# Seven half-block products in place of eight in the last matrix product, with the sums of blocks on POOL and VectorE

## The chip, the cores and the metric

The kernel runs on one core of one Trainium2 chip. The metric is the device time of one execution in microseconds (us); the lower the better. Three runs of the kernel before took 679.25, 680.24 and 680.92 us, median 680.24 us.

## The reference, cut to what matters

Three layers follow each other: attention with keys and values pooled by 8, a soft mixture of experts, and a dense layer with a squared-relu gate. The change touches only the last one, which makes 4608 x 512 outputs from a hidden width of 2048:

```python
def _moe2_ref(x, w_in, w_out, s, b):
    h = x @ w_in                  # 4608x512 @ 512x2048
    r = np.maximum(h, 0.0)
    g = s * (r * r) + b
    return (g @ w_out)            # 4608x2048 @ 2048x512
```

The input x of this layer is c @ slot_out with 32 slots, so the kernel first folds slot_out into w_in (the matrix g_st, 128 rows) and gets h from g_st and the transposed routing weights cT with one matmul of 128 rows.

## The kernel before, in words

All operands are float32. The last product is made in fp32r (one pass of TensorE over a float32 operand) with both factors split into a high and a low part: g_hi*w_hi + g_hi*w_lo + g_lo*w_hi. So each product of blocks is three matmuls.

The tokens go in 9 chunks of 512 (CHUNKS, CH); the hidden width in 16 parts f of 128 (F2C). One chunk and one f is a unit, and there are 144 of them. Per unit:

- TensorE, `hidden`: one matmul of 512 columns into bank 4 or 5 (L1451), issued AHEAD = 3 units early.
- ScalarE, `relu`: bank to r_sb (L845); ScalarE, `high`: g_sb plus b, rounded to fp32r, to r2_hi (L854).
- VectorE, `gate`: s*r*r to g_sb (L1093); VectorE, `low`: g_sb + b - r2_hi to r2_lo (L1099). Both have all their tensor inputs in SBUF.
- TensorE, `products`: for 4 tiles of 128 tokens three matmuls of 512 columns each (L1467, L1468, L1469), accumulated over f in four PSUM banks.

Each engine has its own queue and works it off in order; the order is written out in `units` for ScalarE (L863) and VectorE (L1109), and in `products` (L1454) for TensorE. Waits are on counting semaphores: `low` of unit u lets `products` of unit u start (lo_ready), the end of `products` of u-2 lets `high` of u write its buffer again (unit_done), and `relu` of a unit lets TensorE use that bank again (r_ready). In `units`, ScalarE does relu(f+1), then high(f), and VectorE gate(f+1), then low(f). In the first chunk these queues also make the split of w_out: ScalarE w_hi (L830), VectorE w_lo (L1085), one f each unit; and `keep_g` (L838, L1079). After each chunk four tiles of 128x512 are copied to o_sb (`finish`, L861 and L1107, two on each engine) and stored by SyncE's queue (L644).

POOL (GpSimd) works in the attention stage only: it pools keys and values (L664, L671, L677) and normalises (L684). Its last instruction is a memset at L698.

```python
                    for m in range(MT):
                        toks = slice(P * m, P * (m + 1))
                        acc = acc_bank(odd, m)[:, :]
                        pe.matmul(acc, r2_hi[:, f % 2, toks], w_hi[:, f, :], start=(f == 0), stop=False)
                        pe.matmul(acc, r2_hi[:, f % 2, toks], w_lo[:, f, :], start=False, stop=False)
                        last = pe.matmul(acc, r2_lo[:, f % 2, toks], w_hi[:, f, :], start=False, stop=(f == F2C - 1))
```

Of the kernel before, what the change touches and what calls it, by code (L numbers as in the profile page):

```python
# [18 lines left out]
def pooled_attention_soft_moe_squared_relu_kernel(  # L19
# [55 lines left out]
    AHEAD = 3  # L75
# [18 lines left out]
    assert GL * GH == KEYS and DEN <= BANK and F1 == 2 * BANK and F2 == 4 * BANK and N % CH == 0 and CHUNKS % 2 == 1  # L94
# [3 lines left out]
    with ctx:  # L98
# [15 lines left out]
        early = sb("early", [P, WO, MAT])  # L114
# [42 lines left out]
        r2_hi = sb("r2_hi", [P, 2, CH], F32R)  # L157
        r2_lo = sb("r2_lo", [P, 2, CH], F32R)
# [48 lines left out]
        G_B = (6, 7)  # L207

        def acc_bank(c_odd, m):

            return bank[G_B[m] if c_odd and m < 2 else m]


        TILE_ORDER = (2, 3, 0, 1)
# [86 lines left out]
        h_ready = sem("h_ready")  # L301
        g_ready = sem("g_ready")
        r_ready = sem("r_ready")
# [3 lines left out]
        acc_ready = sem("acc_ready")  # L307
        o_dve = sem("o_dve")
        o_act = sem("o_act")
        stored = [sem(f"stored{m}") for m in range(MT)]  # L310

# [214 lines left out]

        block = ctx.enter_context(nc.Block())

        @block.sync
        def _(sp):
# [103 lines left out]

            for c in range(CHUNKS):
                for n, m in enumerate(TILE_ORDER):
                    sp.wait_ge((o_dve, o_act)[n % 2], 2 * c + n // 2 + 1)
                    sp.dma_start(tile_rows(MT * c + m), o_sb[:, m, :]).then_inc(stored[m], 16)  # L644
            for m in range(MT):
                sp.wait_ge(stored[m], 16 * CHUNKS)

        @block.gpsimd
        def _(pool):
# [48 lines left out]
            pool.memset(hT[:, :, :, :], 0.0).then_inc(hT_zero, 1)  # L698

        @block.scalar  # L700
        def _(act):
# [124 lines left out]
            def split(f):  # L826

                act.wait_ge(wout_in[f // (F2C // WO)], 16)
                wv = early[:, f // (F2C // WO), :].rearrange("p (c f) -> p c f", f=D)
                act.activation(w_hi[:, f, :], wv[:, f % (F2C // WO), :], ACT.Copy).then_inc(w_hi_ready, 1)  # L830

            def keep_part(n):
                act.wait_ge(g_part_psum, n + 1)
                act.activation(g_part[n], bank[n][:, :], ACT.Copy).then_inc(g_part_kept, 1)
# [5 lines left out]
            def relu(n, u, before):  # L840
# [4 lines left out]
                act.activation(r_sb[:, n % 2, :], bank[4 + n % 2][:, :], ACT.Relu).then_inc(r_ready, 1)  # L845

            def high(n, u, c, first):

                act.wait_ge(g_ready, u + 1)
                if n >= 2:  # L850
                    act.wait_ge(unit_done, c * (F2C - 1) + (n - 1))
                elif not first:
                    act.wait_ge((unit_done, acc_ready)[n], c * (F2C - 1, MT)[n])
                act.activation(r2_hi[:, n % 2, :], g_sb[:, n % 2, :], ACT.Identity, bias=sb_col[:, 1:2]).then_inc(hi_ready, 1)  # L854

            def finish(c, odd, second, m):

                act.wait_ge(acc_ready, c * MT + (m + 1))
                if not second:
                    act.wait_ge(stored[m], c * 16)  # L860
                act.activation(o_sb[:, m, :], acc_bank(odd, m)[:, :], ACT.Copy).then_inc(o_act, 1)  # L861

            def units(c, odd, first, second, final):  # L863

                for f in range(F2C):
                    if not (final and f == F2C - 1):
                        relu(f + 1, c * F2C + (f + 1), not first or f)
                    high(f, c * F2C + f, c, first)
                    if first and f + 1 < F2C:
                        split(f + 1)  # L870
                    if first and f < 2:
                        keep_g(2 + f)
                    if not first and f in (0, 2):
                        finish(c - 1, not odd, second, TILE_ORDER[1 + f])

# [7 lines left out]
            relu(0, 0, False)  # L883
            split(0)
            units(0, False, True, False, False)
            units(1, True, False, True, False)
            with act.Fori(2, CHUNKS - 1, 2) as c:
                units(c, False, False, False, False)
                units(c + 1, True, False, False, False)
            units(CHUNKS - 1, False, False, False, True)  # L890
            finish(CHUNKS - 1, False, False, TILE_ORDER[1])
# [3 lines left out]
        def _(dve):  # L895
# [192 lines left out]
            def gate(n, u, before):  # L1088

                dve.wait_ge(r_ready, u + 1)  # L1090
                if before:
                    dve.wait_ge(lo_ready, u - 1)
# [434 lines left out]
```

## Time and profile before

| what | value |
|---|---|
| median of the runs shown | 680.24 us (679.25 to 680.92) |
| the profiled execution | 681.13 us, span 679.3 us |
| TensorE busy | 646.2 us (95%), 5170 matmuls |
| VectorE busy | 369.3 us (54%) |
| ScalarE busy | 325.4 us (48%) |
| POOL busy | 114.8 us (17%) |
| first of the `products` matmuls | 250.8 us |
| last of the `products` matmuls | 674.3 us |

The span is the stretch of the trace from the first to the last instruction; 1.8 us of the profiled execution lie around it. In the trace a matmul's recorded duration includes its way through the array, and matmuls overlap, so what a matmul costs is the distance from its start to the next one's start, not its duration. PE is TensorE's matmuls, PEld its weight loads (each matmul has one, and it runs beside the matmul before). DVE is VectorE, ACT ScalarE, POOL GpSimd.

### The profile page before, as it was taken

To read this page: it belongs to the slowest core of one execution; us is meant where nothing else is said; L and a number is where in the kernel's file an instruction comes from. 1 tells how busy PE (TensorE), PEld (TensorE's weight loads), DVE (VectorE), ACT (ScalarE), POOL (GpSimd) and SP (SyncE) were. 2 spreads that over 40 slices of the span, in tenths; PEclk is the share of its full clock that TensorE was granted. 3 is DMA by queue.
4 is the path that set the end of the run, shared out by engine and by line. 5 is a ranking of instruction groups with operands and counts; after the bars stand their busy time and mean duration, and the time that the engine had idled before them with its cause. 6 is when DMAs were issued, how large, how long until landed. Compare 5 with 4: busy or idle time off the path is not lost.

```text
span 679.3 us, 13164 instructions
## 1 busy us (share of the span) xinstructions
PE 646.2 (95%) x5170; PEld 501.3 (74%) x5170; DVE 369.3 (54%) x610; ACT 325.4 (48%) x599; POOL 114.8 (17%) x117
## 2 busy tenths in 40 slices
PE   6787999989998889999999999999999999999997
PEld 6565677767653248888888888888888888888885
DVE  5757575646344747664454454554544554545543
ACT  1576777767421165654344444443444434443442
POOL 3799777622210000000000000000000000000000
PEclk8899999989999999999999999999999999999999
DMA  9688959573489930010010010000000100100101
GB/s 339 223 264 301 357 201 404 172 295 127 156 311 429 425 166 1 1 52 11 1 62 1 1 62 0 25 37 0 31 31 0 62 0 0 62 1 0 63 0 63
DMA packets 25233, 80.45 MB, mean 118 GB/s; under 512 B 6496, under 2 KB 14688, under 8 KB 22368
## 3 DMA queue, kind: packets, MB, share of 16 engines
q1 hardware_dynamic: 25184, 79.76, 31.5%
q8 instruction: 35, 0.57, 0.4%
q14 instruction: 14, 0.11, 0.1%
HBM read 70.32 MB, written 9.44 MB: 117 GB/s over the span
## 4 chain that ended last, share of the span: by engine, by line
PE 83%; DMA 8%; POOL 3%; DVE 2%; issue 2%; ACT 1%; ACTq 0%; SPq 0%; DVEq 0%; POOLq 0%
PE bank L1467 19%; PE bank L1469 19%; PE bank L1468 19%; PE bank L1451 5%; DMA late<-in_moe_w_dram 4%; PE bank L1318 4%; DMA kvbuf<-in_k_dram 3%; PE bank L1305 2%; PE bank L1242 2%; PE bank L1275 2%; PE bank L1401 2%; PE bank L1348 2%; POOL kvbuf L664 1%; PE bank L1364 1%; PE bank L1201 1%
## 5 line engine op out<-in xcount | busy, mean ns | idle before, releaser
L1467 PE MATMUL bank<-w_hi,r_hi 128*128 128x512 f32 x576 | 224.4, 389 | 1.4 <-DVE r_lo L1099 1.4
L1468 PE MATMUL bank<-w_lo,r_hi 128*128 128x512 f32 x576 | 224.2, 389 | 0.0
L1469 PE MATMUL bank<-w_hi,r_lo 128*128 128x512 f32 x576 | 224.2, 389 | 0.0
L1093 DVE SCALAR_TENSOR_TENSOR win_sb<-win_sb,sb_col 128x512 f32<-128x512 f32 x144 | 108.4, 753 | 197.6 <-ACT win_sb L845 197.5
L845 ACT ACTIVATE win_sb<-bank 128x512 f32<-128x512 f32 x144 | 86.2, 598 | 217.7 <-PE bank L1451 217.7
L1467 PEld LDWEIGHTS bank<-w_hi,r_hi 128*128 128x128 f32 x576 | 108.1, 188 | 24.4 <-DVE r_lo L1099 2.0
L1469 PEld LDWEIGHTS bank<-w_hi,r_lo 128*128 128x128 f32 x576 | 108.1, 188 | 22.4
L1468 PEld LDWEIGHTS bank<-w_lo,r_hi 128*128 128x128 f32 x576 | 108.1, 188 | 22.4
L1099 DVE SCALAR_TENSOR_TENSOR r_lo<-win_sb,sb_col,r_hi 128x512 fp32r<-128x512 f32 x144 | 107.6, 747 | 1.5 <-ACT r_hi L854 1.5
L854 ACT ACTIVATE r_hi<-win_sb,sb_col 128x512 fp32r<-128x512 f32 x144 | 103.3, 717 | 1.6 <-PE bank L1469 1.6
L1451 PE MATMUL bank<-cT,g_st 128*128 (+1 forms) x144 | 56.4, 393 | 0.0
L802 ACT ACTIVATE aT<-bank 72x512 f32<-72x512 f32 x72 | 38.8, 588 | 28.0 <-PE bank L1318 28.0
L684 POOL TENSOR_TENSOR ex<-ex,den 128x576 f32<-128x576 f32 x36 | 41.4, 1150 | 49.4 <-DVE den L998 49.3
L1318 PE MATMUL bank<-ident,ex 128*72 128x128 f32 x288 | 39.6, 281 | 8.0 <-POOL ex L684 5.5
L1318 PEld LDWEIGHTS bank<-ident,ex 128*72 128x72 f32 x288 | 29.5, 116 | 21.5 <-issue 13.7
L948 DVE TENSOR_REDUCE mx<-bank 128x8 f32<-128x576 f32 x36 | 27.2, 756 | 29.6 <-PE bank L1242 24.5
L664 POOL TENSOR_TENSOR kvbuf<-kvbuf 128x768 f32<-128x768 f32 x18 | 32.7, 1817 | 14.1 <-DMA kvbuf<-in_v_dram 8.0
L707 ACT ACTIVATE qT<-bank 128x512 f32<-128x512 f32 x36 | 21.5, 597 | 22.6 <-PE bank L1275 22.4
L1451 PEld LDWEIGHTS bank<-cT,g_st 128*128 128x128 f32 x144 | 27.0, 188 | 6.6 <-DVE g_st L1079 0.8
L1275 PE MATMUL bank<-ident,qbuf 128*128 128x128 f32 x144 | 23.4, 286 | 4.3 <-DMA qbuf<-in_q_dram 3.1
L987 DVE TENSOR_REDUCE den<-ex 128x8 f32<-128x584 f32 x36 | 27.1, 752 | 0.0
L994 DVE TENSOR_TENSOR ex<-bank,mx 128x576 f32<-128x576 f32 x36 | 26.9, 748 | 0.0
(131 smaller groups left out, 552.3 us busy)
## 6 DMA issues: line engine op xcount, KB each, us to landing
early_third<-in_moe_w_dram SPq DMA_DIRECT2D x6, 2048.0 KB, 14.1
kvbuf<-in_k_dram SPq DMA_DIRECT2D x12, 768.0 KB, 5.5
kvbuf<-in_v_dram SPq DMA_DIRECT2D x12, 768.0 KB, 6.2
out_dram<-win_sb SPq DMA_DIRECT2D x36, 256.0 KB, 2.4
qbuf<-in_q_dram SPq DMA_DIRECT2D x8, 1024.0 KB, 9.1
early<-in_moe_w_dram SPq DMA_DIRECT2D x4, 2048.0 KB, 12.4
late<-in_moe_w_dram SPq DMA_DIRECT2D x4, 2048.0 KB, 20.2
win_sb<-in_moe_w_in_dram SPq DMA_DIRECT2D x4, 1024.0 KB, 5.3
```

Of the source, the lines that this page charges most:

```text
L664: pool.tensor_tensor(buf[:, :, 0:ROW // 2], buf[:, :, 0:ROW // 2], buf[:, :, ROW // 2:ROW], ALU.add).then_inc(pool_step, 1)
L684: pool.tensor_tensor(e, e, r, ALU.mult).then_inc(a_ready, 1)
L802: act.activation(aT[:, HB * g:HB * (g + 1), :], bank[A_B[g]][0:KEYS, :].rearrange("p (a g) -> p a g", a=HB), ACT.Copy).then_inc(aT_kept, 1)
L845: act.activation(r_sb[:, n % 2, :], bank[4 + n % 2][:, :], ACT.Relu).then_inc(r_ready, 1)
L854: act.activation(r2_hi[:, n % 2, :], g_sb[:, n % 2, :], ACT.Identity, bias=sb_col[:, 1:2]).then_inc(hi_ready, 1)
L1093: dve.scalar_tensor_tensor(out=g_sb[:, n % 2, :], in0=r_sb[:, n % 2, :], scalar=sb_col[:, 0:1], in1=r_sb[:, n % 2, :], op0=ALU.mult, op1=A ...
L1099: dve.scalar_tensor_tensor(out=r2_lo[:, n % 2, :], in0=g_sb[:, n % 2, :], scalar=sb_col[:, 1:2], in1=r2_hi[:, n % 2, :].bitcast(F32), op0= ...
L1318: last = pe.transpose(bank[A_B[g]][0:KEYS, P * a:P * (a + 1)], ex[:, U % EXR, HB * g + a, 0:KEYS], ident[:, :])
L1451: pe.matmul(bank[4 + f % 2][:, :], g_st[:, P * f:P * (f + 1)], cT[:, bass.ds(c * CH, CH)], start=True, stop=True).then_inc(h_ready, 1)
L1467: pe.matmul(acc, r2_hi[:, f % 2, toks], w_hi[:, f, :], start=(f == 0), stop=False)
L1468: pe.matmul(acc, r2_hi[:, f % 2, toks], w_lo[:, f, :], start=False, stop=False)
L1469: last = pe.matmul(acc, r2_lo[:, f % 2, toks], w_hi[:, f, :], start=False, stop=(f == F2C - 1))
```

## The change

The first 512 tokens are still made as before ("easy" units, with the f in the order FORDER, and the matmuls of `hidden` issued with a lead that grows from 1 to 3 units). The other 4096 tokens go in 16 halves of 256 tokens (HALVES). In a half, the f are taken in pairs k and k+8: a step works on a 2x2 matrix of blocks (two tiles of 128 tokens, two parts of 128 of the hidden width) times a 2x2 matrix of blocks of w_out (two parts f, left and right 256 columns). It needs seven products of 128x128 by 128x256 in place of eight, three matmuls each. A half has 8 steps, so there are 128 steps.

Per step:

- TensorE: two matmuls of 256 columns for h (`hidden`, both into bank 7), issued 5 steps ahead; 21 matmuls of 256 columns (`steps`).
- ScalarE: relu of 512 columns; `add_b` (Identity with bias, 512 columns, in place); `high` (Copy, 896 columns).
- POOL: `token_sums`: three tensor_tensor instructions of 256, 128 and 128 columns, each waiting for the one before; all inputs in SBUF.
- VectorE: `gate` of 512 columns; `low` as a subtraction of 896 columns, both inputs in SBUF; and for 7 of 8 steps a `join` of 256 columns that puts the half before together from the seven sums in PSUM.

The seven sums of a half take 256 columns each (half_bank). ScalarE copies the first to SBUF (keep_p1, once a half). The output is stored as before, one DMA of 256 KB for each 128 tokens.

The block sums of w_out (4 combinations for each of 8 k) are made during the first chunk: POOL makes them (`combos`, 4 instructions of 256 columns for each k), ScalarE rounds them (`combos_high`, 1024 columns, 8 times), and POOL (k < 4) or VectorE (k >= 4) makes the low part (`combos_low`, 1024 columns).

The core of the diff:

```diff
+    AHEAD = 5
+    FORDER = (0, 1, 2, 3, 4, 8, 5, 9, 6, 10, 7, 11, 12, 13, 14, 15)
...
+        def lead(u):
+
+            return 1 if u < 6 else 2 if u < 9 else 3
...
 @block.gpsimd
+            def combos(k):
+
+                if k >= 2:
+                    pool.wait_ge(t_hi_ready, k - 1)
+                    if k - 2 < KP // 2:
+                        pool.wait_ge(t_lo_pool, k - 1)
+                    else:
+                        pool.wait_ge(t_lo_dve, k - 1 - KP // 2)
+                pool.tensor_tensor(t_raw_of(k, T1), raw_block(k, 0, 0), raw_block(k, 0, 1), ALU.subtract).then_inc(t_made, 1)
+                pool.tensor_tensor(t_raw_of(k, T3), raw_block(k, 1, 1), raw_block(k, 0, 1), ALU.add).then_inc(t_made, 1)
+                pool.wait_ge(t_made, COMBOS * k + 1)
+                pool.tensor_tensor(t_raw_of(k, T6), raw_block(k, 1, 1), t_raw_of(k, T1), ALU.subtract).then_inc(t_made, 1)
+                pool.wait_ge(t_made, COMBOS * k + 3)
+                pool.tensor_tensor(t_raw_of(k, T4), raw_block(k, 1, 0), t_raw_of(k, T6), ALU.subtract).then_inc(t_made, 1)
...
+            def token_sums(n, c, k):
+
+                a = a_sb[:, n % ARING, :]
+                pool.wait_ge(gate_ready, c * KP + (k + 1))
+                pool.tensor_tensor(a[:, 4 * P:6 * P].rearrange("p (x f) -> p x f", x=2), a[:, P:3 * P].rearrange("p (x f) -> p x f", x=2),
+                                   a[:, 0:P].unsqueeze(1).to_broadcast([P, 2, P]), ALU.subtract).then_inc(s_made, 1)
+                flip = slice(5 * P, 6 * P)
+                pool.wait_ge(s_made, c * (3 * KP) + (3 * k + 1))
+                pool.tensor_tensor(a[:, 6 * P:7 * P], a[:, P:2 * P], a[:, flip], ALU.add).then_inc(s_made, 1)
+                pool.wait_ge(s_made, c * (3 * KP) + (3 * k + 2))
+                pool.tensor_tensor(a[:, 7 * P:8 * P], a[:, 6 * P:7 * P], a[:, 3 * P:4 * P], ALU.subtract).then_inc(s_made, 1)
...
 @block.scalar
+            def high(n, c, k, first):
+
+                act.wait_ge(s_made, c * (3 * KP) + 3 * (k + 1))
+                if first and k == 1:
+                    act.wait_ge(acc_ready, MT)
+                else:
+                    act.wait_ge(*done_two_before(c, k))
+                act.activation(hi_sb[:, n % 2, :], a_sb[:, n % ARING, P:2 * CH], ACT.Copy).then_inc(hi_ready, 1)
...
+            begun = 1
+            high_at = {3: 0, 5: 1, 7: 2, 8: 3, 9: 4, 11: 5, 14: 6, 15: 7}
+            for u in range(F2C):
+                while begun <= u + lead(u):
+                    relu(begun, begun, bank[4 + begun % 2] if begun < F2C else bank[7], begun >= 2)
+                    begun += 1
+                high_easy(u)
+                if u + 2 >= F2C:
+                    add_b(u + 2, u + 2)
+                if u + 1 < F2C:
+                    split(FORDER[u + 1])
+                if u < 2:
+                    keep_g(2 + u)
+                if u in high_at:
+                    combos_high(high_at[u])
...
 @block.vector
+            def low(n, u):
+
+                dve.wait_ge(hi_ready, u + 1)
+                dve.tensor_tensor(lo_sb[:, n % 2, :], a_sb[:, n % ARING, P:2 * CH], hi_sb[:, n % 2, :].bitcast(F32),
+                                  ALU.subtract).then_inc(lo_ready, 1)
...
+            def steps(c, odd, first, final):
+
+                for k in range(KP):
+                    n = KP * odd + k
+                    low(n, step(c, k))
+                    if not (final and k >= KP - 3):
+                        gate(n + 3, step(c, k) + 3, True)
+                    if first and k in (0, 1):
+                        keep_tile(2 * k + 1)
+                    if not first and k < PARTS7:
+                        join(c - 1, 1 - odd, k)
...
 @block.tensor
+            def products():
+                issued = 3
+                for u in range(F2C):
...
+                    while issued <= u + lead(u) + 2:
+                        hidden_at(issued)
+                        issued += 1
...
+            def steps(c, odd, first, second, final):
...
+                    for at, lhs, rhs_hi, rhs_lo in half_blocks(k):
+                        acc = half_bank(odd, at)
+                        opens = k == 0 and (at == AT1 or at % 2 == 1)
+                        hi, lo = (t[:, n % 2, P * lhs:P * (lhs + 1)] for t in (hi_sb, lo_sb))
+                        pe.matmul(acc, hi, rhs_hi, start=opens, stop=False, skip_group_check=True)
+                        pe.matmul(acc, hi, rhs_lo, start=False, stop=False, skip_group_check=True)
+                        last = pe.matmul(acc, lo, rhs_hi, start=False, stop=(k == KP - 1), skip_group_check=True)
```

## Rows read from the trace of the kernel before

**Rows 1.** The page: slices of TensorE, its granted clock and POOL; the chain.

```profile
PE   6787999989998889999999999999999999999997
POOL 3799777622210000000000000000000000000000
PEclk8899999989999999999999999999999999999999
...
PE bank L1467 19%; PE bank L1469 19%; PE bank L1468 19%; PE bank L1451 5%; DMA late<-in_moe_w_dram 4%; PE bank L1318 4%; DMA kvbuf<-in_k_dram 3%; PE bank L1305 2%; PE bank L1242 2%; PE bank L1275 2%; PE bank L1401 2%; PE bank L1348 2%; POOL kvbuf L664 1%; PE bank L1364 1%; PE bank L1201 1%
```

**Rows 2.** Stretches of the last layer: busy (count) of PE, PEld, DVE, ACT, POOL; clock.

```profile
250.80:298.10 47.30, 47.30 (x209) 39.19 (x210) 33.73 (x50) 26.84 (x48) 0.00 (x0) 1.00 0.00 1
298.10:674.50 376.40, 376.40 (x1662) 311.61 (x1660) 189.10 (x269) 160.90 (x269) 0.00 (x0) 1.00 0.06 23
```

**Rows 3.** Timeline, one unit, hidden to hidden: start, us, engine, line.

```profile
400.97 0.39 PE L1451 MATMUL bank<-cT,g_st 128*128 x1
401.20 0.39 PE L1467 MATMUL bank<-w_hi,r_hi 128*128 128x512 f32 x1
401.40 0.60 ACT L845 ACTIVATE win_sb<-bank 128x512 f32<-128x512 f32 x1 [1.74 <-PE bank L1451]
401.89 0.72 ACT L854 ACTIVATE r_hi<-win_sb,sb_col 128x512 fp32r<-128x512 f32 x1
402.03 0.75 DVE L1093 SCALAR_TENSOR_TENSOR win_sb<-win_sb,sb_col 128x512 f32<-128x512 f32 x1 [1.53 <-ACT win_sb L845]
402.70 0.75 DVE L1099 SCALAR_TENSOR_TENSOR r_lo<-win_sb,sb_col,r_hi 128x512 fp32r<-128x512 f32 x1
...
403.92 0.39 PE L1451 MATMUL bank<-cT,g_st 128*128 x1
```

**Rows 4.** Timeline, runs of matmuls with loads of 128 columns, fp32 (two passes) and transposes.

```profile
174.57 0.53 PEld L1201 LDWEIGHTS bank<-ident 128*128 128x128 f32 x4
174.60 0.69 PE L1201 MATMUL bank<-ident 128*128 128x128 f32 x4
...
211.76 1.97 PE L1409 MATMUL bank<-fold,scratch 128*128 128x32 f32 x16 [0.69 <-ACT scratch L815]
...
247.31 1.88 PE L1446 MATMUL bank<-scratch,fold 128*128 128x512 f32 x4
```

**Rows 5.** Weight loads of the last layer, grouped by line.

```profile
L1468 PEld LDWEIGHTS bank<-w_lo,r_hi 128*128 128x128 f32 x576 | 108.1, 188 | 22.4
```

**Rows 6.** ScalarE and VectorE, groups by line and shape.

```profile
L819 ACT ACTIVATE cT<-bank 128x512 fp32r<-128x512 f32 x8 | 4.8, 597 | 17.0 <-PE bank L1390 17.0
L819 ACT ACTIVATE cT<-bank 128x128 fp32r<-128x128 f32 x4 | 1.1, 276 | 0.0
...
L1065 DVE TENSOR_TENSOR cT<-bank,cT 32x512 fp32r<-32x512 f32 x16 | 11.0, 690 | 11.7 <-ACT cT L819 11.3
L1065 DVE TENSOR_TENSOR cT<-bank,cT 32x128 fp32r<-32x128 f32 x8 | 2.3, 290 | 0.2
```

**Rows 7.** Timeline, start of the first chunk: ScalarE, and the first product.

```profile
248.86 0.72 ACT L854 ACTIVATE r_hi<-win_sb,sb_col 128x512 fp32r<-128x512 f32 x1
249.49 0.61 ACT L830 ACTIVATE w_hi<-early 128x512 fp32r<-128x512 f32 x1
250.00 0.75 DVE L1099 SCALAR_TENSOR_TENSOR r_lo<-win_sb,sb_col,r_hi 128x512 fp32r<-128x512 f32 x1
250.01 0.58 ACT L838 ACTIVATE g_st<-bank 128x512 fp32r<-128x512 f32 x1
...
250.80 0.50 PE L1467 MATMUL bank<-w_hi,r_hi 128*128 128x512 f32 x1 [1.38 <-DVE r_lo L1099]
```

**Rows 8.** POOL, groups by line and shape.

```profile
L671 POOL TENSOR_TENSOR kvbuf<-kvbuf 128x384 f32<-128x384 f32 x18 | 18.0, 1000 | 0.2
L677 POOL TENSOR_TENSOR vp<-kvbuf 128x192 f32<-128x192 f32 x22 | 12.6, 591 | 0.9
```

**Rows 9.** Timeline, a VectorE copy within SBUF beside POOL, and one with POOL idle.

```profile
16.32 1.81 POOL L664 TENSOR_TENSOR kvbuf<-kvbuf 128x768 f32<-128x768 f32 x1 [5.06 <-DMA kvbuf<-in_v_dram]
17.24 1.04 DVE L916 COPY vp<-vp 128x192 f32<-128x192 f32 x1
18.21 0.99 POOL L671 TENSOR_TENSOR kvbuf<-kvbuf 128x384 f32<-128x384 f32 x1
...
196.15 0.23 DVE L1025 COPY sT<-scratch 128x128 f32<-128x128 f32 x1
```

**Rows 10.** VectorE beside POOL, groups by line: all 36 of each.

```profile
L987 DVE TENSOR_REDUCE den<-ex 128x8 f32<-128x584 f32 x36 | 27.1, 752 | 0.0
L994 DVE TENSOR_TENSOR ex<-bank,mx 128x576 f32<-128x576 f32 x36 | 26.9, 748 | 0.0
```

More of the change, by code:

```diff
@@ new lines, in _ @@
+            pool.wait_ge(matrix_used, LAST_SLOT + 1)
+            for i in range(WO):
+                pool.wait_ge(wout_in[i], 16)
+            for k in range(KP):
+                combos(k)
+                if 1 <= k <= KP // 2:
+                    combos_low(k - 1)
+            pool.wait_ge(t_hi_ready, KP)
+            pool.wait_ge(t_lo_dve, KP // 2)
+            for k in range(KP):
+                token_sums(k, 0, k)
+            with pool.Fori(1, HALVES - 1, 2) as c:
+                for x in range(2):
+                    for k in range(KP):
+                        token_sums(KP * x + k, c + x, k)
@@ L700, in _ @@
+            for k in range(KP):
+                token_sums(k, HALVES - 1, k)
         @block.scalar
@@ L838, in keep_g, with relu @@
                 act.activation(g_block(n, slice(0, P)), g_found(n, slice(0, P)), ACT.Copy).then_inc(g_hi, 1)
-            def relu(n, u, before):
+            def relu(n, u, h_bank, before):
                 act.wait_ge(h_ready, u + 1)
@@ L856, in finish @@
-            def finish(c, odd, second, m):
-                act.wait_ge(acc_ready, c * MT + (m + 1))
-                if not second:
[L860 to L874, printed above, removed]
+                a = a_sb[:, n % ARING, 0:CH]
@@ new lines, in keep_tile, with keep_p1 @@
+            def keep_tile(m):
+                act.wait_ge(acc_ready, m + 1)
+                act.activation(o_sb[:, m, :], bank[ACC_B[m]][:, :], ACT.Copy).then_inc(o_act, 1)
+            def keep_p1(c, odd, second):
+                act.wait_ge(half_ready, c * PARTS7 + (AT1 + 1))
+                if not second:
+                    act.wait_ge(joined, c * PARTS7 - 1)
+                act.activation(p1_sb[:, :], half_bank(odd, AT1), ACT.Copy).then_inc(p1_kept, 1)
+            def steps(c, odd, first, second, final):
+                for k in range(KP):
+                    n = KP * odd + k
+                    high(n, c, k, first)
+                    if first and k in (0, 1):
+                        keep_tile(2 * k)
+                    if not first and k == 0:
+                        keep_p1(c - 1, 1 - odd, second)
+                    if not (final and k >= KP - 3):
+                        relu(n + 3, step(c, k) + 3, bank[7], True)
+                    if not (final and k >= KP - 2):
+                        add_b(n + 2, step(c, k) + 2)
@@ L1122, in _ @@
+            def steps(c, odd, first, final):
+                for k in range(KP):
+                    n = KP * odd + k
+                    low(n, step(c, k))
+                    if not (final and k >= KP - 3):
+                        gate(n + 3, step(c, k) + 3, True)
+                    if first and k in (0, 1):
+                        keep_tile(2 * k + 1)
+                    if not first and k < PARTS7:
+                        join(c - 1, 1 - odd, k)
             keep_g(0)
@@ new lines, in hidden_easy, with hidden @@
+            def hidden_easy(u):
+                f = FORDER[u]
+                pe.matmul(bank[4 + u % 2][:, :], g_st[:, P * f:P * (f + 1)], cT[:, 0:CH], start=True, stop=True).then_inc(h_ready, 1)
+            def hidden(c, k):
+                for i in range(2):
+                    f = k + KP * i
+                    last = pe.matmul(bank[7][:, PAIR * i:PAIR * (i + 1)], g_st[:, P * f:P * (f + 1)], cT[:, bass.ds(c * PAIR + CH, PAIR)],
+                                     start=True, stop=True, skip_group_check=True)
+                last.then_inc(h_ready, 1)
```

373 lines of the change are left out of this document (256 added, 117 removed).

## The prediction

> **What bounds the kernel now.** I read the page's slices first: TensorE is at nine tenths or more from about 250 us on, its clock is full there, POOL is empty after the attention stage, and the chain of work runs over the lines of the last product [rows 1]. Then the last layer by stretches: from 298.1 to 674.5 us TensorE is busy the whole time, VectorE 189 of 376 us, ScalarE 161 [rows 2]. The timeline of one unit shows the rhythm: the start of `hidden` comes again after 13 matmuls and 403.92 - 400.97 = 2.95 us, and ScalarE and VectorE wait 1.74 and 1.53 us of it [rows 3]. From the first product at 250.8 to the last at 674.3 us lie 1868 starts, 0.2267 us each. So only what TensorE has to stream sets the time, and a change that takes matmul columns away pays, as long as nothing else becomes slower than TensorE.
>
> **TensorE's part.** The first chunk keeps its matmuls. Behind it stand 8 chunks of 16 units of 13 matmuls: 1664 x 0.2267 = 377.2 us. They become 128 steps of 21 + 2 = 23 matmuls of 256 columns: 2944. The trace has no fp32r matmul of 256 columns. Two rows bound its cost. At 2.4 GHz 512 columns are 213.3 ns, so 13.3 ns are added to each now. If that addition is one per matmul, 256 columns cost 106.7 + 13.3 = 120 ns; if it goes with the columns, 113. Below that, a load of 128 columns can't be repeated faster than 0.113 us: (0.53 - 0.19) / 3 for L1201, and (1.97 - 0.16) / 16 for L1409, where 0.16 is what a recorded matmul holds beyond its pace (0.39 - 0.23) [rows 3, 4]. The upper bound is a load that hides behind nothing, 0.188 us [rows 5], but L1409 shows that loads overlap. Four passes of L1446 take (1.88 - 0.16) / 4 = 0.43 us, two cycles a column and nothing added, so the addition isn't in every matmul; I can't tell which of the two it is and take the dearer, 120 ns. A step is then 23 x 0.120 = 2.76 us, 128 of them 353.3 us: **-23.9 us** (-43.9 at 113 ns).
>
> The Trainium skill (TensorE: Matmul & The Clock Gate, Back-to-back issue gap) has N / 2.4 + 2.5 ns for a matmul, 109 ns at 256 columns, an estimate that would make the 2944 matmuls 321 us. The row of this kernel disagrees at 512 columns (226.7 ns against its 216), so I don't use it.
>
> **What the other engines do in a step.** ScalarE: relu starts 0.49 us before the next instruction [rows 3], `add_b` as L854 takes 0.63 (248.86 to 249.49), a Copy from SBUF 0.52 for 512 columns (249.49 to 250.01) [rows 7] and 0.83 ns for each more ((597 - 276) / 384, [rows 6]), so 0.84 for 896; with keep_p1 once in 8 steps 2.0 us. VectorE: 0.67 for `gate` (402.03 to 402.70, [rows 3]); an element is (690 - 290) / 384 = 1.04 ns [rows 6], so `low` of 896 is 0.67 + 0.40 = 1.07, and a join of 256 is 0.40; with 7 joins in 8 steps 2.1 us. POOL: (1000 - 591) / 192 = 2.13 ns an element and 0.18 us fixed [rows 8], so 0.73 + 0.46 + 0.46 = 1.64 us, and two waits on itself. Each alone fits in 2.76 us. `high` now waits for POOL, and relu and `add_b` are queued behind it; but `add_b` runs two steps ahead of `high`, 5.5 us against POOL's 1.8, so that wait costs nothing while POOL keeps its speed. The chain from the end of TensorE's step k-2 over `high` and `low` to step k is 0.9 + 1.1 us and some 0.2 of signals, hidden behind step k-1 (2.76). The joins and keep_p1 wait for sums that stand one step earlier. The stores are as many and as large as before, 36 of 256 KB, on the same queue. These parts cost nothing as long as VectorE and POOL run at these speeds.
>
> **Whether they do** is the point of the case. At 17.24 us VectorE starts a copy of 192 columns within SBUF while POOL's L664 runs; it is recorded with 1.04 us and ends at 18.28, just after POOL's end at 18.13. The copy of 128 columns with POOL idle takes 0.23 us [rows 9]. So VectorE stood still until POOL's instruction was over. VectorE's instructions with one input, or with one in PSUM, don't: L987 and L994 keep 752 and 748 ns over all 36 [rows 10], POOL or not. No row shows a VectorE instruction with two SBUF inputs beside POOL. That is what `gate` and `low` are, and POOL's sums read SBUF all through. The nearest row is the copy, and I take it that they shut each other out.
>
> Then the two share one path, and a step needs the sum of their times on it. With bare elements: VectorE 1408 x 1.04 = 1.46, POOL 512 x 2.13 = 1.09, together 2.55 us. With whole instructions: 0.67 + 1.07 + 1.64 = 3.38. The copy had its fixed part behind it when POOL let go, so VectorE's doesn't count, and POOL's may; I take the middle, 2.96 us. That is over TensorE's 2.76. 128 x 2.96 = 378.9: **+1.7 us** against 377.2 in place of -23.9; the ends are -23.9 (TensorE's pace) and +55.
>
> The Trainium skill (SBUF — State Buffer, Who interferes with whom) has this as a rule against the change: a VectorE instruction with two SBUF inputs and a GpSimd instruction that reads SBUF exclude each other for their whole length. By it the step is the sum above; without it the step is TensorE's. The trace agrees for the copy (1.04 us); for two inputs no run here shows it.
>
> **The first chunk.** (a) In the code the lead of relu grows at u = 6 and 9. At u = 6 ScalarE must do relu(8) before high(6), but TensorE issues hidden(8) only after products(5). The same holds at u = 7 (relu(9), issued after unit 6), u = 9 (relu(12), after unit 8) and u = 10 (relu(13), after unit 9). Each time TensorE waits for the whole chain: 0.20 from the matmul's streaming to relu (401.40 - 400.97 - 0.23), relu 0.60, L854 0.72, L1099 0.75 [rows 3], 0.05 to start (250.75 to 250.80, [rows 7]): 2.3 us, four times: **+9.3 us**. (b) From the first chunk to the first step: after high(15) ScalarE has add_b and the last combos_high (1024 columns, 0.95), VectorE the last combos_low (1.2), then POOL's sums (1.8), `high` and `low`: 0.63 + 0.63 + 0.95 + 1.2 + 1.8 + 0.9 + 1.1 and 0.5 of signals, 7.7 us after the end of unit 13, of which units 14 and 15 hide 5.9: **+2**. (c) On the shared path: VectorE 48 instructions of 512 and 4 of 1024 columns (28,672 elements), POOL 12,288 elements in 36 instructions. Bare 29.8 + 26.2 = 56, whole 37 + 32.7 = 70, middle 63, against 16 units (47.1) with (a) and (b), 58.4: **+5**, between 0 and +12.
>
> **Sum** against the profiled execution (681.1 us): +1.7 + 9.3 + 2 + 5 = +18, 699.1; that execution is 0.9 over the median, so 698.2, said as **698 us**. The tail (one store after the last join instead of two copies a side) changes by less than 0.5 us and is left at nothing. A measurement of this kernel can tell about 0.3% (2 us) from no change.
>
> **Rivals.**
> 1. Port shared, but only bare elements count, and TensorE sets the step at 2.76: -23.9 + 9.3 + 2 = -12.6, **668 us**; with a step of 2.82 (some turns lost) 676. This is the low end of my own case; I give it 0.13. It decides at a step of (377.2 - 16) / 128 = 2.82 us: below, the change is faster.
> 2. No exclusion for two SBUF inputs, this one on the other side: place, `gate` and `low` beside token_sums; price, -23.9 + 11.3, again 668 us, and **648** if a matmul costs 113 ns. For it: no row has the pair. Against: the copy. 0.22.
> 3. Short matmuls don't pay: from 128 ns on (377.2 / 2944) there is nothing to gain even without any stall, and at 0.188 the loop alone adds 176 us (**868**). Against it: rows 4. 0.02.
> 4. The whole lengths count: a step of 3.38, +55 + 11.3 + 12, **758 us**. In my case's range up to 735; beyond it 0.05.
>
> My own case proper has 0.58, and its own range is 680 to 735. Overall the range is **655 to 735 us**: it takes in rivals 1 and 2 at 120 ns, leaves out their 113 ns, and the ends above. Faster: rivals 1 and 2 nearly whole, 0.34; within 0.3%: 0.05; slower 0.61.
>
> **What the profile after would show.** Start to start of short matmuls within a step: 120 or 113 ns. A step (distance of `hidden` pairs): 2.76 if TensorE sets it, 2.9 to 3.1 if the path does; then TensorE waits each step for `low`, and `gate` and `low` are recorded longer than 0.75 and 1.15 us, with ends at the ends of POOL's instructions. POOL's 128-column sums at 0.46 us, longer if VectorE holds them up. In the first chunk four gaps of 2.3 us at the 7th, 8th, 10th and 11th unit. The prediction is wrong if `gate` keeps 0.75 us beside POOL.

## The result, and the profile after

The kernel became slower: 704.13 us median (698.97 to 706.68, 4 runs) against 679.75 us before, ratio 1.0354 with a 95% interval of 1.0289 to 1.0419. The forecast was 698 us, range 655 to 735, slower with 0.61. The profiled execution took 698.97 us (span 697.2); the sum had been made for 699.1. The other three executions have a lower mean granted clock (0.969 to 0.978 against 0.983) and spans of 702.3 to 704.9 us; more on that below.

The page of the changed kernel, slices, the chain of work that ended last, and the costliest groups (line, engine, operation, tiles, count | busy us, mean ns | idle before, and what ended it):

```profile
POOL 3898776623010057848999999999999999999994
PEclk9899999999998999999999999999999999999999
...
POOL a_sb L799 17%; POOL a_sb L803 16%; POOL a_sb L805 9%; PE bank L1538 4%; PE bank L1462 2%; PE bank L1621 2%; DVE a_sb L1264 2%; PE bank L1525 2%; PE bank L1495 2%; DVE lo_sb L1270 2%; DMA kvbuf<-in_k_dram 2%; PE bank L1642 2%; PE bank L1568 1%; PE bank L1584 1%; PE bank L1421 1%
...
L1276 DVE TENSOR_TENSOR lo_sb<-a_sb,hi_sb 128x896 fp32r<-128x896 f32 x128 | 141.2, 1103 | 89.5 <-ACT hi_sb L1002 86.3
L1002 ACT ACTIVATE hi_sb<-a_sb 128x896 fp32r<-128x896 f32 x128 | 122.1, 954 | 110.8 <-POOL a_sb L805 109.5
L1264 DVE SCALAR_TENSOR_TENSOR a_sb<-r_sb,sb_col 128x512 f32<-128x512 f32 x144 | 140.0, 972 | 11.4 <-ACT r_sb L980 11.3
L805 POOL TENSOR_TENSOR a_sb<-a_sb 128x128 f32<-128x128 f32 x128 | 125.9, 984 | 10.0
L799 POOL TENSOR_TENSOR a_sb<-a_sb 128x256 f32<-128x256 f32 x128 | 122.1, 954 | 5.1 <-DVE t_late L1257 4.9
L803 POOL TENSOR_TENSOR a_sb<-a_sb 128x128 f32<-128x128 f32 x128 | 109.0, 851 | 10.0
```

POOL is at nine tenths where it was idle [rows 1], and the chain runs over its three sums for 42% of the span, where it ran over the products before. The last sum (L805) has as many columns as the one before it (L803), 128, and both take about twice the 0.46 us they need: over a third of POOL's busy time is waiting inside an instruction (349 us in the loop here, 213 in experiment 6 for the same sums). `gate` (L1264) was 0.75 us [rows 3] and is 0.97. `low` (L1276) keeps its plain length, 1.10 us in the mean and 1.18 at most, so between these two it is POOL that stands. ScalarE's `high` waits 109.5 us for POOL, VectorE's `low` 86.3 us for `high`.

The stretches of the last layer, first chunk and steps (busy and count of PE, PEld, DVE, ACT, POOL; clock):

```profile
251.20:319.50 68.30, 52.33 (x215) 40.20 (x216) 55.58 (x55) 36.31 (x59) 41.84 (x36) 0.98 0.00 1
319.50:693.20 373.70, 370.04 (x2936) 356.53 (x2934) 285.49 (x363) 262.69 (x394) 348.87 (x379) 1.00 0.06 24
```

Against [rows 2]: the loop takes 373.7 us in place of 376.4 to 377.2, 2.92 us a step. The first chunk takes 68.3 us in place of 47.3. The rest of the span is as before within 1 us. So the whole loss of these two executions (18 us) lies in the first chunk, 21.0 us, and the loop, which streams 12% fewer columns, gave back some 3 us of it, 1% of its time.

The timeline of about one step of the changed kernel (start, us, engine, line), without the product's matmuls:

```profile
463.43 0.74 POOL L799 TENSOR_TENSOR a_sb<-a_sb 128x256 f32<-128x256 f32 x1
463.59 0.95 ACT L1002 ACTIVATE hi_sb<-a_sb 128x896 fp32r<-128x896 f32 x1 [1.33 <-POOL a_sb L805]
464.25 0.46 POOL L803 TENSOR_TENSOR a_sb<-a_sb 128x128 f32<-128x128 f32 x1
464.44 0.59 ACT L980 ACTIVATE r_sb<-bank 128x512 f32<-128x512 f32 x1
464.57 1.09 DVE L1276 TENSOR_TENSOR lo_sb<-a_sb,hi_sb 128x896 fp32r<-128x896 f32 x1 [1.09 <-ACT hi_sb L1002]
464.79 1.19 POOL L805 TENSOR_TENSOR a_sb<-a_sb 128x128 f32<-128x128 f32 x1
464.92 0.71 ACT L986 ACTIVATE a_sb<-a_sb,sb_col 128x512 f32<-128x512 f32 x1
465.58 0.95 DVE L1264 SCALAR_TENSOR_TENSOR a_sb<-r_sb,sb_col 128x512 f32<-128x512 f32 x1
465.94 1.19 POOL L799 TENSOR_TENSOR a_sb<-a_sb 128x256 f32<-128x256 f32 x1
466.10 0.95 ACT L1002 ACTIVATE hi_sb<-a_sb 128x896 fp32r<-128x896 f32 x1 [0.46 <-POOL a_sb L805]
```

Here the turns can be read. `low` starts at 464.57, when POOL's L803 has 0.14 us to go, and takes its plain 1.09 us: the ends of two instructions can overlap a little. L805 is issued at 464.79 and ends at 465.98, 1.19 us for 0.46 us of work; taken back from its end, it stood until about 465.5, when `low` was nearly through (465.66). `gate` is issued at 465.58 behind it and takes 0.95 in place of 0.75. L799 then waits for `gate`: 1.19 for 0.74. Both engines look busy, but for much of the time only one of them works.

The matmuls of a step start every 120 ns; the timeline of the fastest kernel below has them undisturbed.

### The profile page after: what moved, and what is told of

Same layout as the page of the kernel before. It is cut to its first block, busy times and chain, and to the rows that moved or that the text cites. A ratio compares the mean times of both kernels' runs of the same rounds, so it can differ in the third digit from the quotient of the medians.

```text
span 697.2 us, 17047 instructions
## 1 busy us (share of the span) xinstructions
PE 649.5 (93%) x6450; PEld 549.8 (79%) x6450; DVE 489.5 (70%) x710; ACT 437.0 (63%) x735; POOL 511.9 (73%) x537
## 4 chain that ended last, share of the span: by engine, by line
POOL 44%; PE 27%; issue 12%; DVE 9%; ACT 3%; DMA 3%; POOLq 1%; DVEq 0%; ACTq 0%
POOL a_sb L799 17%; POOL a_sb L803 16%; POOL a_sb L805 9%; PE bank L1538 4%; PE bank L1462 2%; PE bank L1621 2%; DVE a_sb L1264 2%; PE bank L1525 2%; PE bank L1495 2%; DVE lo_sb L1270 2%; DMA kvbuf<-in_k_dram 2%; PE bank L1642 2%; PE bank L1568 1%; PE bank L1584 1%; PE bank L1421 1%
## 5 line engine op out<-in xcount | busy, mean ns | idle before, releaser
L1276 DVE TENSOR_TENSOR lo_sb<-a_sb,hi_sb 128x896 fp32r<-128x896 f32 x128 | 141.2, 1103 | 89.5 <-ACT hi_sb L1002 86.3
L1002 ACT ACTIVATE hi_sb<-a_sb 128x896 fp32r<-128x896 f32 x128 | 122.1, 954 | 110.8 <-POOL a_sb L805 109.5
L1264 DVE SCALAR_TENSOR_TENSOR a_sb<-r_sb,sb_col 128x512 f32<-128x512 f32 x144 | 140.0, 972 | 11.4 <-ACT r_sb L980 11.3
L805 POOL TENSOR_TENSOR a_sb<-a_sb 128x128 f32<-128x128 f32 x128 | 125.9, 984 | 10.0
L799 POOL TENSOR_TENSOR a_sb<-a_sb 128x256 f32<-128x256 f32 x128 | 122.1, 954 | 5.1 <-DVE t_late L1257 4.9
L1749 PE MATMUL bank<-w_hi,hi_sb 128*128 128x256 f32 x384 | 114.5, 298 | 3.7 <-issue 1.0
L803 POOL TENSOR_TENSOR a_sb<-a_sb 128x128 f32<-128x128 f32 x128 | 109.0, 851 | 10.0
L1750 PE MATMUL bank<-w_lo,hi_sb 128*128 128x256 f32 x384 | 108.6, 283 | 0.0
L1751 PE MATMUL bank<-w_hi,lo_sb 128*128 128x256 f32 x384 | 108.5, 283 | 0.0
L1750 PE MATMUL bank<-t_early,hi_sb 128*128 128x256 f32 x256 | 72.4, 283 | 0.0
L1749 PE MATMUL bank<-t_late,hi_sb 128*128 128x256 f32 x256 | 72.4, 283 | 0.0
L1749 PE MATMUL bank<-t_early,hi_sb 128*128 128x256 f32 x256 | 72.4, 283 | 0.0
L1750 PE MATMUL bank<-t_late,hi_sb 128*128 128x256 f32 x256 | 72.4, 283 | 0.0
```

Source lines behind the costliest of these rows:

```text
L799: pool.tensor_tensor(a[:, 4 * P:6 * P].rearrange("p (x f) -> p x f", x=2), a[:, P:3 * P].rearrange("p (x f) -> p x f", x=2), a[:, 0:P].uns ...
L803: pool.tensor_tensor(a[:, 6 * P:7 * P], a[:, P:2 * P], a[:, flip], ALU.add).then_inc(s_made, 1)
L805: pool.tensor_tensor(a[:, 7 * P:8 * P], a[:, 6 * P:7 * P], a[:, 3 * P:4 * P], ALU.subtract).then_inc(s_made, 1)
L1002: act.activation(hi_sb[:, n % 2, :], a_sb[:, n % ARING, P:2 * CH], ACT.Copy).then_inc(hi_ready, 1)
L1264: dve.scalar_tensor_tensor(out=a_sb[:, n % ARING, 0:CH], in0=r_sb[:, n % 2, :], scalar=sb_col[:, 0:1], in1=r_sb[:, n % 2, :], op0=ALU.mult ...
L1276: dve.tensor_tensor(lo_sb[:, n % 2, :], a_sb[:, n % ARING, P:2 * CH], hi_sb[:, n % 2, :].bitcast(F32), ALU.subtract).then_inc(lo_ready, 1)
```

## The experiments

All are edits of the changed kernel. "Port theory" is short for the theory of the forecast: VectorE's instructions with two SBUF inputs and POOL's reads of SBUF exclude each other; the "shared path" is what they take turns on. Where parts of an execution are given (chunk, loop, step), they are of the one profiled execution of that version.

**1. POOL writes, but reads next to nothing.** It leaves out the block sums of tokens.

```diff
-                pool.tensor_tensor(a[:, 4 * P:6 * P]..., ALU.subtract).then_inc(s_made, 1)
...
+                pool.tensor_tensor(a[:, 4 * P:4 * P + 1], spare[:, 0:1], spare[:, 0:1], ALU.add)
+                for lo, hi in ((4 * P + 1, 6 * P), (6 * P, 7 * P), (7 * P, 8 * P)):
+                    pool.memset(a[:, lo:hi], 0.0).then_inc(s_made, 1)
```

> Leaves out the three block sums of tokens in each step: POOL writes zeros there (an add of one column, then three memsets of 255, 128 and 128 columns), so it still stands between add_b and high, but reads next to nothing. The pace of the matmuls, the joins, gate and low are unchanged. Port theory (VectorE's two-input instructions and POOL's reads exclude each other): gate falls from 0.97 to 0.75 us, low from 1.10 to 1.09, a step is TensorE's own 23 x 0.120 = 2.76 us instead of 2.93, and the kernel is 128 x 0.17 = 22 us faster than the changed one, about 682 us (ratio to before 1.00). The first chunk keeps its 68 us. Rival (POOL's chain of three instructions is simply long, and high waits for it): the step also falls, but gate keeps 0.97 us. Rival (gate is slow because of its new addresses or its ring of four): gate stays at 0.97 and the step falls little.

Measured: 681.73 us, ratio to before 1.0014 (0.9989 to 1.0038). The waits of its loop (engine, line waited for: us in total, times, longest), and a `gate` beside POOL from its timeline:

```profile
ACT hi_sb L1000 <- PE bank L1749: 83.7, 122, 1.6
ACT hi_sb L1000 <- POOL a_sb L802: 1.0, 1, 1.0
...
449.55 0.75 DVE L1262 SCALAR_TENSOR_TENSOR a_sb<-r_sb,sb_col 128x512 f32<-128x512 f32 x1
449.68 0.66 POOL L800 TENSOR_TENSOR a_sb<-spare 128x1 f32<-128x1 f32 x1 [1.57 <-ACT a_sb L984]
```

The loop takes 352.1 us, 2.75 a step: TensorE's own pace. `high` waits for TensorE instead of POOL, and `gate` is back at 0.75 us. POOL's add of a single column, issued 0.13 us into `gate`, takes 0.66 us, although it has nothing to do but read one column: it ends at 450.34, just after `gate` at 450.30. One step on it is issued 0.40 us into `gate`, takes 0.39 us and again ends with it (453.10 and 453.05). The first chunk took 72.2 us and not the 68 expected, with some 17 us at half clock in it (the last section is on that). The rivals fall: a `gate` slow by its address or its ring would have stayed slow. That POOL was also quicker here (memsets) is a second difference; experiments 3 and 6 don't have it.

**2. One more POOL read in each step.**

```diff
+                pool.tensor_tensor(spare[:, :], a[:, P:2 * P], a[:, 2 * P:3 * P], ALU.add)
                 pool.tensor_tensor(a[:, 7 * P:8 * P], a[:, 6 * P:7 * P], a[:, 3 * P:4 * P], ALU.subtract).then_inc(s_made, 1)
```

> One more POOL instruction in each step: an add of 128 columns with both inputs in SBUF, into a spare buffer, ahead of the last sum (0.27 us of elements, 0.46 us whole). Port theory: the step goes from 2.93 to between 3.2 and 3.4 us, all of it, since the path is full; 35 to 59 us over 128 steps, 735 to 763 us, and the part that shows tells how much of a POOL instruction shuts VectorE out. If POOL's chain of signals is the bound instead of the path, it is also 0.46 more, 3.39. If neither binds (TensorE at 2.76 does, with stray waits), the step grows by less than 0.1 us.

Measured: 758.75 us, ratio 1.1172 (1.1123 to 1.1220). The loop takes 429.5 us, 3.36 a step: 0.44 more for an instruction of 0.46 us. Its `high` waits 167.4 us for POOL:

```profile
L1004 ACT ACTIVATE hi_sb<-a_sb 128x896 fp32r<-128x896 f32 x128 | 122.0, 953 | 167.4 <-POOL a_sb L807 167.4
```

So one more POOL instruction costs nearly its whole length, the fixed 0.18 us included, and not just its elements (0.27). The run alone can't tell the path from a long chain through POOL, as its expectation says.

**3. `gate` with one input in PSUM.** relu(h) * h equals relu(h) squared, so the output is the same.

```diff
-                                         in1=r_sb[:, n % 2, :], op0=ALU.mult, op1=ALU.mult).then_inc(g_ready, 1)
+                                         in1=h_bank[:, :], op0=ALU.mult, op1=ALU.mult).then_inc(g_ready, 1)
...
-                        pe.wait_ge(r_ready, step(c, k) + AHEAD)
+                        pe.wait_ge(g_ready, step(c, k) + AHEAD)
```

> gate multiplies relu(h) with h itself, read from its PSUM bank, in place of relu(h) twice; the value is the same, and only one input is in SBUF. TensorE may refill the bank only after gate instead of after relu. Port theory: gate stands at 0.75 us beside POOL and POOL's sums lose what gate held them up; the shared path then carries low 1.07 and POOL 1.64 = 2.71 us a step, so the step falls from 2.93 to TensorE's 2.76 to 2.82, 14 to 22 us over the loop, and some 3 to 6 us more in the first chunk: 677 to 687 us. A cost against it: hidden now waits for gate of the step before, which ends about when TensorE's step does, up to 0.1 us a step, 13 us. Rival (the path is not what counts, only the length of the chain add_b, sums, high, low): no change in the step, 704 us, or slower by the later bank.

Measured: 701.49 us, ratio 1.0299 (1.0231 to 1.0367); the interval overlaps that of the changed kernel. Groups and waits of its loop:

```profile
L1264 DVE SCALAR_TENSOR_TENSOR a_sb<-r_sb,sb_col,bank 128x512 f32<-128x512 f32 x144 | 106.5, 740 | 16.5 <-ACT r_sb L980 16.5
L799 POOL TENSOR_TENSOR a_sb<-a_sb 128x256 f32<-128x256 f32 x128 | 95.0, 742 | 147.8 <-ACT a_sb L986 142.3 <-DVE t_late L1257 5.5
L805 POOL TENSOR_TENSOR a_sb<-a_sb 128x128 f32<-128x128 f32 x128 | 60.8, 475 | 10.0
...
ACT hi_sb L1002 <- PE bank L1751: 101.4, 115, 1.3
PEld bank L1678 <- DVE a_sb L1264: 9.9, 43, 0.3
```

The instructions did exactly what the port theory says: `gate` 0.74 us, POOL's sums 0.74 and 0.46 to 0.48 us, POOL idle for 148 us. And the step didn't get shorter, 2.96 us: the time is that of the rival, not the 677 to 687 us of the port theory. (The first chunk took 66.2 us, 2 less.) The expectation had the new wait at 0.1 us a step at most. From the end of the products of one step a chain runs over high (0.95), low (1.09), gate (0.74) and the signals between them to the bank that hidden wants, 2.9 us, more than TensorE's 2.76. The trace puts only 9.9 us on that wait (43 times), of the 26 us by which this loop (378.4 us) is over TensorE's own 352; what the rest is, it doesn't name. Whether the wait was all was left to experiments 6 and 7.

**4. hidden issued early enough in the first chunk.**

```diff
-                    while issued <= u + lead(u) + 2:
+                    while issued <= u + lead(u + 2) + 2:
```

> In the first chunk TensorE issues the matmuls of hidden two units earlier where the lead grows (lead(u + 2) in place of lead(u)), so that relu(8), relu(9), relu(12) and relu(13) find their bank filled. If the order is the cause of the gaps at units 6, 7, 9 and 10 (3.3, 3.9, 3.9 and 2.9 us over a unit's 2.95), the gaps there fall by 2.3 us each, 9 us in all: about 695 us. If they are mostly the shared path (combos on POOL beside gate, low and the split of w_out), the gaps shift and less than 4 us is won: 700 us or more. The loop stays at 2.93 us a step.

Measured: 693.21 us, ratio 1.0218 (1.0140 to 1.0295), some 9 us below the changed kernel as a ratio (1.0354 - 1.0218), though the two intervals just touch. In the profiled execution the first chunk takes 63.5 us in place of 68.3, and the loop stays at 374.0; 2.3 us of its gain lie ahead of the chunk, where nothing was changed. The gaps before the 7th, 8th, 9th, 10th and 11th unit, 3.3, 3.9, 1.8, 3.9 and 2.9 us over the usual 2.95 in the changed kernel, are 3.3, 2.8, 0.3, 2.3 and 1.7. The 2.8 before the 8th is the clock: the twelve products of the 7th unit are at half clock, 0.43 us apart, and no gap follows them. So the gap of the order is gone there, but the first one stands as it was. The order was a cause, but not of the whole. What else holds the first gap is in the trace of the changed kernel:

```profile
267.48 2.84 POOL L793 TENSOR_TENSOR t_early<-a_sb,t_early 128x1024 fp32r<-128x1024 f32 x1
267.99 2.88 DVE L1253 TENSOR_TENSOR w_lo<-early,w_hi 128x512 fp32r<-128x512 f32 x1
```

VectorE's split of w_out (L1253, two SBUF inputs), 0.69 us in the kernel before, is issued 0.5 us into POOL's low part of 1024 columns, stands behind it and takes 2.88 us. In this experiment the same pair takes 2.85 and 2.89 us; the next gate comes late by it, relu waits 1.94 us for that gate, and high stands behind relu in ScalarE's queue.

**5. POOL reads nothing in the first chunk.** It leaves out the block sums of w_out and four of their low parts (zeros are written).

```diff
-                pool.tensor_tensor(t_raw_of(k, T1), raw_block(k, 0, 0), raw_block(k, 0, 1), ALU.subtract).then_inc(t_made, 1)
...
+                for x in range(2):
+                    pool.memset(a_sb[:, 2 * (k % 2) + x, CH:2 * CH], 0.0).then_inc(t_made, 2)
```

> Leaves out the block sums of w_out and the four low parts that POOL makes: POOL writes zeros there (memsets of 512 and 1024 columns); ScalarE's and VectorE's parts of them and all waits stay. So in the first chunk POOL reads nothing beside VectorE. If the shared path has the larger share of the first chunk's 21 us over before, the chunk falls from 68.3 to about 59 us (the four order gaps of 2.3 us and the crossing of 2 to 3 us stay): 694 us. If the order alone makes the gaps, the chunk stays at 66 us or more: 702 us. The loop stays at 2.93 us a step.

Measured: 693.88 us, ratio 1.0195 (1.0152 to 1.0238), again 10 us below. 2.8 of the 4.8 us between the two profiled executions lie ahead of the chunk. The split of w_out (median of its 16 instructions) falls from 1.21 to 0.68 us. The timeline at the first of the gaps:

```profile
266.41 0.60 ACT L976 ACTIVATE r_sb<-bank 128x512 f32<-128x512 f32 x1 [2.35 <-PE bank L1668]
266.90 0.71 ACT L989 ACTIVATE hi_sb<-a_sb,sb_col 128x512 fp32r<-128x512 f32 x1
268.51 0.50 PE L1698 MATMUL bank<-w_hi,hi_sb 128*128 128x512 f32 x1 [2.14 <-DVE lo_sb L1266]
```

With POOL out of the way the gaps stand where the order puts them: relu waits for hidden, then high and low follow, and the unit is 5.25 us long in place of 2.95. That is the 2.3 us of the forecast. Two of the four show it (before the 7th and the 10th unit); the other two are 4.0 us, because the clock fell there. The profiled chunk took 66.4 us, far from the 59 expected, with four stretches of 3.4 us at half clock in it; the changed kernel's profiled execution had one. By the chunk it is the rival's 66, by the time (694 us) the port theory. An estimate without the clock settles it: each such stretch costs some 1.7 us (units of 4.69 us for 2.95 here), so the chunk would be 59.6 us, and the changed kernel's 66.6. Of the 21 us over before, POOL's reads then cost about 7, the clock 1.7, and the order and the crossing the 12 that are left.

**6. Everything that helps at once.** Experiments 3 and 4, and hidden moved away from the end of the step:

```diff
+                        if at == AT6 and not (first and k == 0):
+                            if k + 4 < KP:
+                                pe.wait_ge(g_ready, step(c, k) + 4)
+                                hidden(c, k + 4)
+                            elif not final:
+                                pe.wait_ge(g_ready, step(c, k) + 4)
+                                hidden(c + 1, k + 4 - KP)
...
-                    if k + AHEAD < KP:
-                        pe.wait_ge(r_ready, step(c, k) + AHEAD)
-                        hidden(c, k + AHEAD)
```

> Three things together: gate with h from PSUM, the earlier hidden of the first chunk, and hidden moved from the end of a step to behind the second of its seven blocks in the next step, so that TensorE no longer meets gate's end (in the run with gate from PSUM alone, hidden waited for gate 43 times and high for TensorE nearly every step, while POOL's sums were back at 0.46 us). Port theory, completed by that wait: nothing holds TensorE any more; the shared path carries low 1.07 and POOL 1.64 = 2.7 us, so a step is 2.76 to 2.80 us, the loop 353 to 358 us in place of 374, the first chunk about 62 us in place of 68: 670 to 678 us, which is below the kernel before (ratio 0.985 to 0.995). If the wait for gate's bank was not what kept the step at 2.96, it stays above 2.90 and the time above 690 us.

Measured: 668.88 us, ratio **0.9856** (0.9831 to 0.9882). Stretches, the waits of its loop, and six of its matmuls:

```profile
250.00:308.60 58.60, 51.40 (x215) 40.40 (x216) 51.97 (x56) 37.91 (x61) 42.62 (x38) 0.97 0.01 5
308.60:662.30 353.70, 353.70 (x2936) 353.54 (x2934) 278.84 (x362) 272.10 (x393) 212.63 (x378) 1.00 0.07 25
...
POOL a_sb L799 <- ACT a_sb L986: 107.7, 115, 1.2
ACT hi_sb L1002 <- PE bank L1751: 71.9, 120, 1.6
...
450.47 0.28 PE L1751 MATMUL bank<-w_hi,lo_sb 128*128 128x256 f32 x1
450.59 0.28 PE L1749 MATMUL bank<-w_hi,hi_sb 128*128 128x256 f32 x1
450.71 0.28 PE L1750 MATMUL bank<-w_lo,hi_sb 128*128 128x256 f32 x1
450.83 0.28 PE L1751 MATMUL bank<-w_hi,lo_sb 128*128 128x256 f32 x1
450.95 0.28 PE L1749 MATMUL bank<-t_early,hi_sb 128*128 128x256 f32 x1
451.07 0.28 PE L1750 MATMUL bank<-t_early,hi_sb 128*128 128x256 f32 x1
```

TensorE is busy for all 353.7 us of the loop, 2.76 a step, and a matmul of 256 columns starts every 120 ns. POOL is recorded with 213 us in place of 349 on the same sums; ScalarE waits for TensorE, and POOL for ScalarE. The exclusion isn't gone: `low`, which keeps two SBUF inputs, is now recorded with 1.26 us (1.10 in the changed kernel), behind POOL's last sum; TensorE's 2.76 us hide it. The time is 1 us below the range of 670 to 678, with a chunk of 58.6 us in place of 62.

**7. Is it the place of hidden alone?** The same move in the changed kernel, with `gate` as it was (the waits are on r_ready).

> The changed kernel with hidden alone moved behind the second block of the next step; gate still takes both inputs from SBUF. Port theory: the shared path (low, gate and POOL's sums) sets the step, so it stays at 2.93 us, at most 0.05 either way, and the time at that of the changed kernel, 700 to 706 us. If the place of hidden is what matters in the combined run, the step falls to 2.80 here too and the time to about 687 us.

Measured: 702.95 us, ratio 1.0335 (1.0300 to 1.0370); 2.92 us a step, `gate` 0.97 us: the move alone gains nothing. So for the loop the two edits work only together (experiment 4's edit leaves it at 374.0 us): `gate` from PSUM frees the shared path but makes the bank late, and the move frees the bank.

**8. The first chunk again.** On top of 6, the rounding of w_out's block sums goes earlier in two queues:

```diff
-            high_at = {3: 0, 5: 1, 7: 2, 8: 3, 9: 4, 11: 5, 14: 6, 15: 7}
+            high_at = {2: 0, 4: 1, 6: 2, 8: 3, 9: 4, 11: 5, 13: 6, 14: 7}
...
-            low_at = {9: 4, 12: 5, 14: 6, 15: 7}
+            low_at = {9: 4, 11: 5, 13: 6, 14: 7}
```

> The combined version (668.9 us) with the rounding of w_out's block sums moved one to two units earlier in ScalarE's and VectorE's queues of the first chunk (after units 2, 4, 6, 8, 9, 11, 13, 14 in place of 3, 5, 7, 8, 9, 11, 14, 15). In the combined run POOL stood idle 8.1 us before its first low part, ScalarE then waited 2.2 and 3.0 us for POOL's sums at the 5th and 6th, a gap of 3.4 us before one product followed, and at the end of the chunk the first step came 6.4 us after the last product in place of 3.0. If POOL's late start is the cause, the gap goes and the crossing shrinks: the chunk falls from 58.6 to 53 to 56 us and the time to 663 to 667 us. If the shared path is full in this stretch anyway, the wait only moves to another unit and the time stays within 2 us of 668.9.

Measured: **664.59 us**, ratio **0.9788** (0.9753 to 0.9824), the fastest version. Its stretches:

```profile
249.30:305.70 56.40, 51.07 (x216) 39.08 (x217) 52.62 (x56) 37.72 (x60) 42.02 (x36) 1.00 0.01 5
305.70:657.90 352.20, 352.20 (x2936) 352.12 (x2934) 279.06 (x361) 272.10 (x393) 212.72 (x378) 1.00 0.07 25
```

From the start of the last unit's products to the first step it is now 4.0 us in place of 6.4 (the expectation calls this "after the last product"; a unit is 2.95), and the unit of 6.3 us is gone. But the last unit but one has become 4.4 us, from 3.0, so part of the wait only moved. The chunk is 2.2 us shorter, just outside the 53 to 56 expected, and the loop 1.5. Most of that is the clock and not the order by itself: the profiled execution of experiment 6 had one stretch at half clock at the start of its chunk (its first unit took 4.7 us, here 3.3) and one right behind the crossing, this one had none. The time meets the expectation (663 to 667 us); how much of it the new order gives by fewer falls of the clock is not shown. Some 9 us over the 47.3 of before are left in the chunk, and no run takes them apart.

## Why the prediction was right

- **TensorE's price.** 120 ns for 256 columns was the dearer of two readings, an addition of 13.3 ns on each matmul rather than on its columns. It is 120 ns (experiment 6). The 109 ns of the Trainium skill (TensorE: Matmul & The Clock Gate, Back-to-back issue gap) is not reached.
- **VectorE and POOL exclude each other.** Taken over from one copy [rows 9] to instructions with two SBUF inputs, and this is what the trace after shows: L805 with 1.19 us for 0.46, L799 with 1.19 for 0.74, `gate` with 0.95 for 0.75. The rows carried this less far than the prediction says: the copy has one input, so its own sentence that VectorE's instructions with one input don't stand behind POOL doesn't hold for the copy, and nothing in the rows led from the copy to two inputs. From the rows alone that step was a guess; the runs bore it out. One sign was missed too: `low` was to be longer than 1.15 us and kept 1.10; there POOL stood instead. Experiments 1 and 3 take the reads or the second SBUF input away and the durations fall back. An input in PSUM is enough to be free of it, as [rows 10] had it. That is the rule of the Trainium skill (SBUF — State Buffer, Who interferes with whom). The runs here agree with it for two inputs: gate 0.97 us beside POOL's reads, 0.74 with one of them in PSUM.
- **Its size.** The middle between bare elements and whole lengths, 2.96 us a step, was a choice without a reason of its own, and that 2.92 was measured (373.7 against 378.9 us) is luck in the size. The added instruction of experiment 2 costs 0.44 of its 0.46 us. Taken as whole lengths the changed kernel's step would be 3.38, and it is 2.92, so parts of the two engines' times do overlap, as the 0.14 us of L803 and `low` above.
- **The order in the first chunk.** The four gaps stand at the four units named, and experiment 5 shows their 2.3 us bare, twice. In the changed kernel they are 2.9 to 3.9 us, and two more, of 1.2 and 1.8 us before the 5th and the 9th unit, were not named.
- **What was too small:** the first chunk. Forecast 9.3 + 2 + 5 = 16.3 us over the 47.3 of before, measured 21.0. The crossing was 2.4 (2 forecast). The rest is the term for the shared path, +5, for which experiment 5 leaves about 7 (an estimate), and the clock, 1.7, for which no term stood. The term spread the two engines' times evenly over the chunk; the trace shows single long stands, as the 2.88 us of the split of w_out, which pass their delay on to gate, relu and high.
- The sum of 699.1 us for the profiled execution met 698.97 partly by luck: the loop came out 5 us better and the chunk 5 us worse. The median of the changed kernel, 704 us, is 6 us over the forecast of 698.
- **Rivals.** 1 and 2 wanted a step at TensorE's pace, 2.76 to 2.82 us; 2.92 refutes them, and the longer `gate` refutes 2 in its cause as well. That pace came only once POOL's reads (experiment 1), or `gate`'s second SBUF input together with the wait for the bank (6), were gone. 3 is refuted by the 120 ns, 4 by 2.92 us a step.

## What to carry to other kernels

Taking matmul columns away pays only what the other engines' new work leaves of the gain; before moving elementwise work to POOL, look for VectorE instructions with two SBUF inputs beside it, and give them one input from PSUM where the algebra allows it. Opening one wait can close another of the same length: when an edit frees its instructions (durations fall, the engine idles) and the time stays, read who waits for whom again before dropping it. An engine that looks 90% busy may be waiting inside its instructions; compare the durations of instructions of the same size.

## What was not expected of the hardware

**The clock in the first chunk.** Behind some of the waits between dense products the granted clock is at half (1.2 GHz) for a while. The changed kernel around the gap before the 7th unit, by stretches (the first is the wait, the clock is the third number from the right):

```profile
270.50:273.90 3.40, 0.86 (x4) 0.38 (x2) 3.38 (x4) 1.73 (x3) 3.32 (x4) 1.00 0.01 2
273.97:277.38 3.41, 3.05 (x7) 2.47 (x8) 1.44 (x2) 0.00 (x0) 0.90 (x1) 0.50 0.00 0
...
274.33 0.79 PE L1702 MATMUL bank<-w_hi,hi_sb 128*128 128x512 f32 x1 [2.97 <-DVE lo_sb L1270]
275.35 0.63 PE L1704 MATMUL bank<-w_hi,lo_sb 128*128 128x512 f32 x1
275.78 0.63 PE L1702 MATMUL bank<-w_hi,hi_sb 128*128 128x512 f32 x1
```

At 1.2 GHz the matmuls start 0.43 us apart in place of 0.227, so a stretch full of products loses some 1.7 us. The profiled executions of the versions here had none (experiment 8) to about five such stretches in this chunk (1 and 7). That is where the spread within the changed kernel seems to come from: its spans are 697.2, 702.3, 702.3 and 704.9 us at mean clocks of 0.983, 0.976, 0.978 and 0.969, in nearly that order. That the gaps cause the fall is read from their order in the traces and was not tested by itself, and it isn't the whole rule: in this same execution a longer gap (product starts 4.24 us apart, against 3.58 here) was followed by no fall, while in experiment 5 one of 2.75 us was. The fastest version, whose longest extra wait in the chunk was some 1.5 us, had no such stretch in its profiled execution.
